# Attention steps with whole 128-wide tiles, two rank products, the v products' result in another PSUM bank, rows one step later, and the early expert tile woven into the last steps

## What is computed

```python
# attention: batch 4, heads 8, seq 576, head_dim 64
scores = scale * q @ k.T
thresh = max(scores) - tau                     # of each row
scores = where(scores >= thresh, scores, -1e9)
attn = exp(scores - max); attn /= attn.sum() + 1e-9
x = attn @ v                                   # 2304 tokens x 512
# experts: E = 8, D = 512, F = 1024
logits = x @ w_gate + modality_bias[modality_id]
e = argmax(logits); gate = softmax(logits)[e]
x = gate * (relu(x @ w1[e]) @ w2[e])
# feed-forward: 512 -> 2048 -> 512, h * tanh(softplus(h))
out = g(x @ w_in) @ w_out
```

## Time and profile before

| | |
|---|---|
| median of 3 runs | 998.81 us (998.07 to 999.24) |
| profiled execution, its own time | 998.59 us |
| its span, first to last instruction | 996.9 us |
| TensorE busy | 964.4 us, 97% |
| VectorE busy | 675.2 us, 68% |
| ScalarE busy | 503.5 us, 51% |
| GpSimd busy | 484.3 us, 49% |
| granted TensorE clock, mean | 0.996 |

### The profile page before, as it was taken

The page is one execution under the profiler, slowest core; times in us unless marked ns, Lnnn a source line. Parts: engine busy times, 40 slices in busy tenths (PEclk is TensorE's granted clock), DMA queues, the critical chain, the costliest instruction groups (busy, mean ns, idle before and its releaser), DMA issues.

```text
span 996.9 us, 17681 instructions
## 1 busy us (share of the span) xinstructions
PE 964.4 (97%) x6176; PEld 803.5 (81%) x6177; DVE 675.2 (68%) x1223; ACT 503.5 (51%) x971; POOL 484.3 (49%) x575
## 2 busy tenths in 40 slices
PE   6999999999998999999999989999999999999996
PEld 4777777777776878888887778988889889898995
DVE  5788888978885451111115489978878888888784
ACT  3656666666665242222225455555555545455552
POOL 3222225765432156400000066786786776777885
PEclk9999999999999999999999999999999999999999
DMA  2212227222111437311124300000100100000000
GB/s 99 73 49 70 76 84 267 101 73 90 64 68 54 161 110 274 100 45 45 44 75 150 142 32 1 33 33 1 33 32 1 33 32 1 33 1 1 33 1 32
DMA packets 21785, 65.85 MB, mean 66 GB/s; under 512 B 3536, under 2 KB 3536, under 8 KB 21456
## 3 DMA queue, kind: packets, MB, share of 16 engines
q1 hardware_dynamic: 14368, 39.90, 11.7%
q0 software_dynamic: 4896, 20.00, 5.6%
q10 hardware_dynamic: 2448, 5.01, 1.8%
HBM read 46.63 MB, written 18.27 MB: 65 GB/s over the span
## 4 chain that ended last, share of the span: by engine, by line
PE 85%; POOL 5%; DVE 4%; issue 3%; ACT 1%; DMA 0%; ACTq 0%; DVEq 0%; POOLq 0%; SPq 0%
PE psum L416 6%; PE psum L1302 5%; PE psum L1286 5%; PE psum L1288 5%; PE psum L1287 5%; PE psum L1304 5%; PE psum L1303 5%; PE psum L373 4%; PE psum L388 4%; PE psum L1000 3%; PE psum L973 3%; PE psum L1002 3%; PE psum L1001 3%; PE psum L975 3%; PE psum L974 3%
## 5 line engine op out<-in xcount | busy, mean ns | idle before, releaser
L1400 DVE RECIPROCAL rr<-rr 128x384 f32<-128x384 f32 x96 | 244.1, 2543 | 9.3 <-ACT rr L1348 9.3
L497 ACT ACTIVATE prob<-ssb,smin 128x576 f32<-128x576 f32 x144 | 111.6, 776 | 105.4 <-DVE ssb L600 105.4
L1236 POOL TENSOR_TENSOR uu<-uu,ex 128x384 f32<-128x384 f32 x96 | 97.2, 1013 | 105.0 <-ACT uu L1342 104.5
L600 DVE TENSOR_SCALAR_CACHE_REDUCE ssb<-psum,tauk 128x576 f32<-128x576 f32 x144 | 112.6, 816 | 47.1 <-PE psum L376 39.2
L1286 PE MATMUL psum<-x2T_hi,w_in_hi 128*128 128x384 f32 x384 | 131.0, 341 | 1.7 <-DVE x2T_lo L1418 1.7
L294 POOL TENSOR_TENSOR limit<-smin,margin 128x2 f32<-128x2 f32 (+1 forms) x80 | 57.6, 720 | 148.1 <-DVE ssb L600 147.7
L1288 PE MATMUL psum<-x2T_hi,w_in_lo 128*128 128x384 f32 x384 | 129.5, 337 | 0.0
L1287 PE MATMUL psum<-x2T_lo,w_in_hi 128*128 128x384 f32 x384 | 129.1, 336 | 0.0
L1052 DVE TENSOR_TENSOR hT_lo<-psum,hT_hi 128x512 fp32r<-128x512 f32 x38 | 26.3, 691 | 146.9 <-ACT hT_hi L1029 146.9
L1302 PE MATMUL psum<-w_hi,g_hi 128*128 128x512 f32 x288 | 114.8, 399 | 6.5 <-POOL g_lo L1247 6.5
L1304 PE MATMUL psum<-w_hi,g_lo 128*128 128x512 f32 x288 | 114.3, 397 | 0.0
(11 more groups left out here) (206 smaller groups left out, 2213.3 us busy)
## 6 DMA issues: line engine op xcount, KB each, us to landing
qk<-in_qk_dram SPq DMA_DIRECT2D x16, 640.0 KB, 4.1
vsb<-in_v_dram SPq DMA_DIRECT2D x16, 512.0 KB, 3.5
xrow<-xs ACTq DMA_DIRECT2D x17, 288.0 KB, 2.8
ys<-ysb SPq DMA_DIRECT2D x19, 257.0 KB, 3.1
stage<-in_w_in_dram POOLq DMA_DIRECT2D x16, 256.0 KB, 3.6
wa<-in_wa_dram SPq DMA_DIRECT2D x8, 512.0 KB, 6.8
wb<-in_wb_dram SPq DMA_DIRECT2D x8, 512.0 KB, 10.5
xs<-zrow SPq DMA_DIRECT2D x11, 288.0 KB, 2.4
```

The source lines that it names most:

```text
L497: act.activation(prob[:, n % 3, cols], ssb[:, w, cols], ACT.Exp, bias=smin[:, w, h:h + 1], scale=-1.0).then_inc(exp_done, 1)
L600: dve.tensor_scalar(ssb[:, w, h * S:(h + 1) * S].rearrange("p (a q) -> p a q", a=2), b_bank if h else a_bank, factor, BIG, ALU.mult, ALU.m ...
L1400: dve.reciprocal(rr[:, n % 4], rr[:, n % 4]).then_inc(r_done, 1)
```

## The change

- The constants: routing begins one step later (ROUTE = PER + 4). There is one more constant tile, zeros beside the identity, so that a 128-wide matrix that moves partitions 64 up (`shift`) is a view of it.
- PSUM: the result of `pv` moves from bank 7 to bank 6, beside the transposed rest. Rows, ranks and moved sums stay in bank 7.
- `turn`: the rest of tile 4 is transposed 128 wide; it waits also for the copy of the previous `pv` result, since both are in one bank.
- `pv`: the last products of tile 4 use all 128 partitions. It waits for both copies before its first product, and no longer for x and the ranks.
- `rows_out`: always 128 rows; the moved sums come from a product with 128-wide weights. The waits for x and the ranks are here now.
- `ranks`: two products in place of six; VectorE first makes a sum over a window of tiles (`ahead_in_p`).
- Order of TensorE in a step: scores of c, products of c-3, rows of c-4, transposes of c-2.
- `evacuate`: the 128 columns of the rest first, then the 1024.
- The loops end at step 79; the rest of attention and the first early tile are in a new written-out order on TensorE, ScalarE and VectorE. `up_half` can run other work between its products.

The core of the diff:

```diff
-ROUTE, RANK = PER + 3, 7
+ROUTE, RANK = PER + 4, 7
...
-    turn_bank, rest_bank = psum[:, 4:6, :], psum[:, 6, 0:P]
-    ot_bank, rank_bank = psum[:, 7, 0:P], psum[:, 7, P:P + (TT + 1) * E]
+    turn_bank, rest_bank, ot_bank = psum[:, 4:6, :], psum[:, 6, 0:P], psum[:, 6, P:2 * P]
+    rank_bank, moved = psum[:, 7, 0:(TT + 1) * E], psum[:, 7, (TT + 1) * E:(TT + 1) * E + 1]
...                                                   turn
-            if full:
-                pe.transpose(rest_bank, prob[:, w, QT * P:QT * P + P], ident[:]).then_inc(turned, 1)
-            else:
-                pe.transpose(rest_bank[0:REM, :], prob[:, w, QT * P:S], ident[:]).then_inc(turned, 1)
+                pe.wait_ge(ot_out, n)
+            pe.transpose(rest_bank, prob[:, w, QT * P:QT * P + P], ident[:]).then_inc(turned, 1)
...                                                   pv
             pe.wait_ge(main_out, n + 1)
+            pe.wait_ge(rest_out, n + 1)
             if n >= 1:
                 pe.wait_ge(ot_out, n)
-                pe.wait_ge(x_done, norms(n))
...                                                   rows_out
+            if n >= 1:
+                pe.wait_ge(x_done, norms(n))
...
-                last = pe.matmul(moved, ident[D:P, D:P], rsum[D:P, p % 2, 2 * QT:TPP], start=True, stop=True)
+                last = pe.matmul(moved, t["shift"], rsum[:, p % 2, 2 * QT:TPP], start=True, stop=True)
...                                                   ranks
-            for tt in range(TT):
-                last = pe.matmul(rank_bank[:, (tt + 1) * E:], ones[:],
-                                 oh[:, tt, :].unsqueeze(1).to_broadcast([P, TT - tt, E]),
-                                 start=False, stop=(tt == TT - 1))
+            pe.matmul(rank_bank, ones[:], ahead_in_p.rearrange("p t e -> p (t e)"),
+                      start=False, stop=True).then_inc(rank_done, 1)
...                                                   order on TensorE
-        for c in range(NS + 1):
-            if c < NS:
-                scores(c)
+        for c in range(NS):
+            scores(c)
             if c >= 3:
                 pv(c - 3)
+            if c >= 4:
+                rows_out(c - 4)
             if c >= 2:
                 turn(c - 2)
-            if c >= 3:
-                rows_out(c - 3)
...
+        pv(NS - 3)
+        pe.wait_ge(copied, units(NS - 1))
+        turn_x(0)
+        rows_out(NS - 4)
+        turn(NS - 2)
+        pe.wait_ge(copied, units(NS))
+        up_half(0, 0, 0)
         pv(NS - 2)
-        pe.wait_ge(copied, units(NS))
-        turn_x(0)
+        rows_out(NS - 3)
         turn(NS - 1)
         rows_out(NS - 2)
-        up_half(0, 0, 0)
-        pv(NS - 1)
-        pe.wait_ge(main_out, NS)
-        up_half(0, 1, 0)
-        rows_out(NS - 1)
+        up_half(0, 1, 0, {1: lambda: pv(NS - 1), KT - 1: lambda: rows_out(NS - 1)})
         turn_x(1)
...                                                   evacuate
             if n % TT < QT:
+                act.copy(pt[:, w, 2 * QT * P:], rest_bank).then_inc(rest_out, 1)
                 act.copy(pt[:, w, 0:2 * QT * P], turn_bank.rearrange("p a q -> p (a q)")).then_inc(main_out, 1)
-                act.copy(pt[:, w, 2 * QT * P:], rest_bank).then_inc(rest_out, 1)
...                                                   the last steps on ScalarE
-        copy_out(NS - 2)
+        copy_out(NS - 3)
         x_hi(0)
         gate_of(0)
+        evacuate(NS - 2)
+        relu(0, 0)
+        copy_out(NS - 2)
         evacuate(NS - 1)
-        relu(0, 0)
         copy_out(NS - 1)
...                                                   choose on VectorE
             elif k == 6:
-                dve.tensor_tensor(oh[:, 0:TT], chosen[:].unsqueeze(2).to_broadcast(wide), evalid[:],
-                                  ALU.is_equal).then_inc(oh_done, 1)
+                window = bass.AP(oh[:].tensor, oh[:].offset, [list(oh[:].ap[0]), [E, TT + 1], [1, E], [E, TT]])
+                dve.tensor_reduce(ahead_in_p, window, AX.X, ALU.add).then_inc(oh_done, 1)
...                                                   the last steps on VectorE
-        invert(NS - 2)
-        normalise(NS - 2)
+        probs(NS - 1, 0)
         x_lo(0)
-        h_lo(0, 0)
-        invert(NS - 1)
-        normalise(NS - 1)
+        for n in (NS - 4, NS - 2, NS - 1):
+            invert(n)
+            normalise(n)
         for k in range(RANK):
             choose(B - 1, k)
+            if k == 2:
+                h_lo(0, 0)
```

More of the change, by code:

```diff
@@ L440, in rows_out @@
             pe.wait_ge(ot_out, n + 1)
+            if n >= 1:
+                pe.wait_ge(x_done, norms(n))
+            b, k = divmod(n + 3 - ROUTE - RANK, PER)
+            if k == 0 and b >= 0:
+                pe.wait_ge(ranks_read, b + 1)
             c = (tt % 2) * 2 * HW
-            m = P if tt < QT else REM
-            last = pe.matmul(row_bank[0:m, c:c + 2 * HW], otsb[:, n % 2, 0:m],
+            last = pe.matmul(row_bank[:, c:c + 2 * HW], otsb[:, n % 2],
                              wx[:, p % HP].rearrange("p h c -> p (h c)"), start=True, stop=True)
@@ L521, in gate_exps @@
             act.activation(le[:], le[:], ACT.Exp).then_inc(lexp_done, 1)
-        for c in range(NS + 1):
-            if c < NS:
-                exps(c, 0)
+        for c in range(NS):
+            exps(c, 0)
             if c >= 3:
                 copy_out(c - 3)
-            if c < NS and c % TT < QT:
+            if c % TT < QT:
                 exps(c, 1)
@@ L644, in normalise @@
             else:
-                step(dve.reciprocal(rinv[0:REM, TPP:TPP + 1], moved))
+                step(dve.reciprocal(rinv[0:REM, TPP:TPP + 1], moved[0:REM]))
                 r = rinv[0:REM, 2 * QT:2 * TT].unsqueeze(2)
@@ L741, in count_full @@
                 note(dve.tensor_reduce(done_early[:, 0:1], full[:], AX.X, ALU.add))
-        for c in range(NS + 1):
-            if c < NS:
-                copy_scores(c, 0)
-                if c % TT < QT:
-                    copy_scores(c, 1)
-            if 3 <= c:
-                invert(c - 3)
-            if 1 <= c < NS + 1:
+        for c in range(NS):
+            copy_scores(c, 0)
+            if c % TT < QT:
+                copy_scores(c, 1)
+            if 4 <= c:
+                invert(c - 4)
+            if 1 <= c:
                 probs(c - 1, 0)
@@ L753, in vector @@
                     probs(c - 1, 1)
-            if 3 <= c:
-                normalise(c - 3)
+            if 4 <= c:
+                normalise(c - 4)
             if c == ROUTE // 2:
@@ L962, in turn_x, with up_half @@
             last.then_inc(x_turned, 1)
-        def up_half(i, half, split):
+        def up_half(i, half, split, between={}):
             c = slice(half * 512, (half + 1) * 512)
@@ L972, in up_half @@
                     turn_h(i, 0)
+                if k in between:
+                    between[k]()
                 pe.matmul(h_bank[:, half, :], xT_hi[:, k], w1h[:, k, c], start=(k == 0), stop=False)
@@ L1469, in build @@
         sb = placer(nc, base)
+        wide = sb("ident", [P, P + REM])
         t = {"sem": sem, "psum": ctx.enter_context(nc.psum_tensor("psum", [P, 8, 512], F32)),
-             "ident": sb("ident", [P, P]), "ltri": sb("ltri", [P, P]), "ones": sb("ones", [P, P]),
+             "ident": wide[:, 0:P], "shift": wide[:, D:D + P], "zcols": wide[:, P:], "ltri": sb("ltri", [P, P]), "ones": sb("ones", [P, P]),
              "slots": sb("slots", [P, B * TT], U32), "out_ids": sb("out_ids", [P, 2, CT], U32),
```

31 lines of the change are left out of this document (13 added, 18 removed).

## The result

The changed kernel takes 1003.93 us (median of 5 runs, 1003.34 to 1006.42), the kernel before 998.53 in the same session (997.87 to 999.24): ratio 1.0054, 95% interval 1.004 to 1.0069. It is slower by 5.4 us. The profiled execution took 1005.9, with 1004.3 between first and last instruction, and is thus one of the two longer of the five (1005.9, 1006.42; the others 1003.34 to 1003.93).

What follows compares the result with a forecast made beforehand. TensorE was taken as the bound, with ScalarE's copies right behind it. Steps +6.9, first steps -0.25, ranks -2.4, VectorE +0.2 and last steps +0.9 sum to +5.3 on 998.59: 1003.9 us, range 995 to 1008.

Steps and rivals of the forecast that it cites:

- Copies, 1.54 from T: Attention steps: from the last transpose (T) to the products with v, ScalarE's two copies need 0.31 + 1.18 + 0.05 us.
- The first rival: Attention steps: ScalarE's copies do not bind, so the whole gain comes, 987 us (985 to 990); chance 0.14.
- The pair, +0.46: Five attention steps of a pair of heads: waits of 1.05 us less 0.59 saved, over 15 pairs +6.9.
- Steps 0 and 4: Steps opened by scores of tiles 0 (full) and 4 (short): TensorE waits 0.17 and 0.37 us for copies.
- Step 2: Step opened by tile 2's scores, with tile 4's products: new length without waits 1.17 + 2.15 = 3.32 us.
- Step 3: Step opened by tile 3's scores: tile 0's products wait 0.34 us, and the single-column product gives back 0.20.
- step 1: Step with tile 4's transposes: a wait of 0.17 us, and 0.17 saved by ending the change after the 64-wide transpose.
- Whole tiles, -0.59: Per pair of heads, savings around tile 4: 0.17 + 0.17 + 0.45 - 0.20 us.
- Ranks, -2.4 in the steps: Rank products on TensorE's path: 1.26 us falls to 0.42, three times in the steps; VectorE pays +0.2 in all.
- The last steps, +0.9: From the last scores to the first down product: 20.45 becomes 22.1 us, +1.7, less 0.8 for the ranks.
- VectorE did not take over: Rival: in tile 4's shortened step VectorE's copies of scores come late, 0.3 us per pair more, 1008; chance 0.06.
- The paid-off case: Rival: smaller waits pay for the saving, per pair 0.1 to 0.2 us above the old, 998.6 us; chance 0.10.

Runs made afterwards that it cites:

- half copy: Changed kernel with ScalarE copying only 512 of the 1024 columns from the third tile on; last scores at 302.42, total 1022.21 us with other token routing.
- rows last: Changed kernel with the transposes before the rows again, rows still of the step four back; 1001.04 us, ratio 1.0015 to the kernel before.
- Whole tiles alone: Kernel before with all tiles 128 wide, order, banks and waits otherwise as before; 997.01 us, ratio 0.9978.
- ranks alone: Kernel before with two rank products and VectorE's reduction over a window of tiles; 997.96 us, ratio 0.9995.
- h first: Changed kernel with VectorE taking the low part of h before it divides the last rows; 1002.39 us, ratio 1.0032 to the kernel before.
- ranks and tiles: Kernel before with both 128-wide tiles and two rank products, nothing else; 996.92 us, ratio 0.9979.
- bank: Kernel before with the v products' result in bank 6, small copy first and waits moved to fit, order of rows as before; 1006.34 us, ratio 1.0074.
- GpSimd held back: Changed kernel with GpSimd waiting before the third w_in piece until VectorE has split two experts' second matrix; 1002.40 us, ratio 1.0023 to the kernel before.

## Why the prediction was right, and where its steps were not

The time (1003.9) and the mechanism were right: TensorE gives up work and waits for ScalarE's copies, and this outweighs the saving. The medians differ by 5.4 where the sum had 5.3. That agreement is better than the working deserves, as the terms show.

*Copies, 1.54 from T.* Right in each step shown above: 0.31 from T to the first copy, 1.18 for both, 0.05 to the products. The copies in turned order follow each other as I took it; the bound of 1.28 did not come. The first rival (copies do not bind) fell, by the half copy.

*The pair, +0.46.* Measured +0.47. Steps 0 and 4 agree to 0.01. Step 2 took 3.40 for 3.32. Some 0.04 of it is that the rest tile's transpose waits for the copy in its bank, in the changed kernel's timeline:

```profile
173.39 0.19 ACT L512 COPY otsb<-psum 128x64 f32<-128x64 f32 x1
173.72 0.30 PE L398 MATMUL psum<-ident,prob 128*128 128x128 f32 x1
```

Step 3 took 4.22 for 4.29. ScalarE's copies began 3.60 after step 2's scores, as worked out, so that what step 2 lost was not waited for again (0.30 for 0.34), and the single-column product costs 0.14, not 0.20 (from the rows to the transposes 0.39, 176.77 to 177.16, against 0.25 in a step without it). The bank was the part that I costed at nothing, without saying so; alone it made step 1 0.19 and step 2 0.05 longer, and the moved rows hide most of it. Beside rows last, the moved rows are thus a gain in steps 1 and 2 (3.576 for 3.776, 3.399 for 3.708) and a loss in the other three, and I saw only the loss.

*Whole tiles, -0.59.* One term stood for the wrong reason: the 0.17 of the 64-wide transpose. Whole tiles alone left step 1 at 3.572. What the 0.62 of the earlier trace rows held was the rows' wait for the copy of the products, and it went because the rows moved a step later. The sum came out right since both edits are in the change. The Trainium skill, "TensorEngine Tiling (Array Packing)", section "Key Properties", has a drain at each change of mode: the holes of 0.09 in the kernel before agree, but here removing one bought nothing, since another wait lay over it.

*Ranks, -2.4 in the steps.* 0.86 for each, right in size (0.84), but in the experiment with ranks alone only 0.43 of three times 0.86 were left at the last scores. In the changed kernel step 52 grows by 0.92 in the same way, where I had counted 0.2 for all that VectorE pays: a VectorE copy of 5 columns, 0.17 in the kernel before, takes 1.28 beside GpSimd's subtraction, and the rest tile's transpose then waits for a late copy:

```profile
210.49 1.26 POOL L333 TENSOR_TENSOR w_lo<-wb,w_hi 128x512 fp32r<-128x512 f32 x1
210.50 1.28 DVE L698 COPY x<-ids 128x5 f32<-128x5 f32 x1
...
213.66 0.30 PE L398 MATMUL psum<-ident,prob 128*128 128x128 f32 x1 [0.80 <-ACT otsb L512]
```

In the changed kernel the last scores come 4.77 later; the sum had 4.45 (6.9 - 0.25 - 2.4 + 0.2).

*The last steps, +0.9.* Measured 0.0. The scatter came 0.48 after the last scores, where the working has it about 0.1 before them (7.7 - 2.9 - 4.89), but the load followed it by 3.75 and not by 4.89; so it landed sooner (turning at 7.08, not 7.7), and the first down product came at 21.35, not 22.1; that it waits for h was right (1.58 for 1.7). This term was too large by 0.9.

*Missing.* The 2.6 at tile 4. I followed the shift only to the end of the early tile and wrote that it goes to the end. In the profiled execution the parts are 4.77 + 0.0 + 2.6 = 7.4, against 5.3. Three of the five runs are 2 to 3 us shorter than the profiled one. No trace shows whether they lack just this loss, but the other kernels' traces point that way: where tile 4 to 5 takes 16.66 to 16.93 (ranks alone, rows last, h first) the traced execution is the kernel's longest, 2.4 to 4.5 above its median, and where it takes 14.19 to 14.22 (before, tiles, ranks and tiles, bank) it is at most 0.7 above it. If so, the steps and the last steps make 4.8 of the medians' 5.4, and 0.6 has no place yet; the sum had 5.3 because its last steps were 0.9 too large and its steps 0.3 too small. That the totals agree to 0.1 is then partly luck; the mechanism is not.

*The rivals.* VectorE did not take over in the ordinary steps of the changed kernel. It did in step 52, where with a routing operation on top the copies of scores came late, as that rival has it; once, for 0.92. In the kernel with whole tiles alone it did, for 0.14 in step 3, through the normalised x and not through the copies of scores that I had named. The paid-off case fell too: only the wait in step 3 is smaller than worked out, by 0.04.

## What to carry to other kernels

When an engine is busy for 97% of the span, first work out the slack of the engine that feeds it, step by step: here 0.25 and 0.05 us decided over a saving of 0.59. A filler instruction between a result and its next user may be the cover of a copy; moving it is no free edit, and neither is moving a result into a bank that another engine still empties. Follow a shift past the part that is changed, to the next place where two engines' loads meet.

## What the runs showed of the hardware

**VectorE and GpSimd slow each other.** Two cases in attention are shown above: 1.20 and 1.28 for VectorE operations of 40 and 5 columns that take 0.18 and 0.17 otherwise. The third case is in the expert tiles. VectorE subtracts 128x1024 to get the low part of the second expert matrix, GpSimd 128x512 for the feed-forward weights. GpSimd and VectorE of the changed kernel, with the product that waits:

```profile
373.32 3.84 DVE L1109 TENSOR_TENSOR w_lo<-wb,w_hi 128x1024 fp32r<-128x1024 f32 x2
...
373.95 2.13 POOL L919 TENSOR_TENSOR w_in_lo<-stage,w_in_hi 128x512 fp32r<-128x512 f32 x1
...
377.72 1.29 POOL L919 TENSOR_TENSOR w_in_lo<-stage,w_in_hi 128x512 fp32r<-128x512 f32 x1
377.91 0.77 PE L999 MATMUL psum<-w_hi,hT_hi 128*128 128x512 f32 x1 [2.72 <-DVE hT_lo L1051]
```

GpSimd's subtraction takes 2.13 beside VectorE's and 1.29 when VectorE doesn't subtract; single ones of VectorE's four take 1.63 to 2.33, the shortest in the kernel before 1.23. The low part of h is queued behind them. The Trainium skill, "SBUF — State Buffer", section "SBUF: two separate sides", holds that the two share a port pair which one of them holds for a whole instruction; VectorE takes it with two SBUF inputs, against a GpSimd instruction that reads SBUF, or in a 2-port mode. The lengthened times agree with taking turns (1.20 and 1.28 beside GpSimd's 1.26); that it is a port, and in which mode the copy of 5 columns ran, no run here shows. In the kernel before the product waited 1.46 at this place, and in the changed one 2.72. The first of the four subtractions took 1.23 there and 1.82 here: the change moved the two loads against each other. The ranks alone did it too, in the traced execution (1.45 and a wait of 2.37).

**A wait of TensorE can cost more than its own length.** Windows of the changed kernel (length; busy time and count of PE, PEld, DVE, ACT, POOL; granted clock, DMA share, GB/s), first the wait, then what follows it:

```profile
374.60:377.90 3.30, 0.59 (x5) 0.37 (x4) 3.30 (x4) 1.17 (x3) 2.92 (x4) 0.94 0.37 131
377.90:381.10 3.20, 3.19 (x10) 2.67 (x11) 0.53 (x2) 0.59 (x1) 2.82 (x4) 0.53 0.60 146
```

The same place of the kernel before:

```profile
369.80:371.90 2.10, 0.64 (x6) 0.42 (x4) 2.10 (x3) 1.17 (x3) 2.02 (x2) 1.00 0.68 233
371.90:375.10 3.20, 3.20 (x16) 2.65 (x17) 1.12 (x2) 0.59 (x1) 2.82 (x4) 1.00 0.42 108
```

After the wait of 2.72 the granted clock is 0.53, near the lower level of 1.2 GHz, and a pass of 512 columns comes every 0.43 us instead of 0.233: ten records in the 3.2 us, where the kernel before has sixteen. Of the 2.6 us lost at tile 4, 1.26 are the longer wait (2.72 - 1.46), and the other 1.4 are this stretch. The low level is also found after a wait of 1.6 us, in the kernel with GpSimd held back, whose early tile went from 14.79 to 16.35:

```profile
330.00:336.40 6.40, 4.81 (x44) 3.76 (x43) 2.84 (x12) 2.13 (x6) 0.00 (x0) 1.00 0.00 0
336.40:340.50 4.10, 4.10 (x14) 3.30 (x15) 3.02 (x10) 0.72 (x2) 0.00 (x0) 0.58 0.27 72
```

The changed kernel has nearly the same wait there (1.58) and the same TensorE work before it, and its clock stayed at 1.00:

```profile
330.00:336.40 6.40, 4.83 (x43) 3.67 (x43) 2.85 (x12) 2.23 (x6) 0.00 (x0) 1.00 0.00 0
336.40:340.50 4.10, 4.09 (x22) 3.47 (x23) 3.22 (x12) 0.72 (x2) 0.00 (x0) 1.00 0.28 72
```

So whether a wait of this length costs 1.6 us more or nothing was not settled by what TensorE did before it. In the kept traces, of the waits of TensorE in the early and the expert tiles, all five of 2.37 to 3.62 us (change, ranks alone, rows last, half the copy, h first) have the low level behind them, one of the four of 1.58 and 1.59, and none of the five of 1.43 to 1.47. Later (564 to 609 us) each of the 13 traces has one wait of 1.67 to 1.69, never with the low level behind it, and one of 3.92 to 3.94, always with it. That one wait of 1.6 can cost this and the next not would fit the two groups among the changed kernel's runs, but it is an argument; the shorter runs left no trace, and the mean clocks on record (0.996 and 0.994 for the two longer runs, 0.994, 0.997 and 0.996 for the others) do not sort them.
